# Mixing stage: 128-row transform tiles, an earlier split of the second weight, and a new order of norms and cosines

## What is computed

```python
def _moe_ref(x, w_ch1, w_ch2):
    X = np.fft.fft(x, axis=1)
    X = np.fft.fft(X, axis=2)
    mixed = np.real(X).astype(np.float32)
    u = x + mixed
    mu = np.mean(u, axis=-1, keepdims=True)
    var = np.mean((u - mu) ** 2, axis=-1, keepdims=True)
    un = (u - mu) / np.sqrt(var + 1e-06)
    ch = np.maximum(un @ w_ch1, 0.0) @ w_ch2
    return (u + ch).astype(np.float32)
```

## Time and profile before

| | |
|---|---|
| median of 3 runs | 956.68 us (956.54 to 957.53) |
| the profiled execution: its own time | 955.61 us |
| its span, first to last instruction | 953.5 us |
| mean granted TensorE clock | 0.912 |
| busy: PE, DVE, ACT, POOL | 90%, 49%, 33%, 21% |
| attention | to about 278 us |
| mixing | about 278 to 668 us |
| gated network | from about 671 us |

### The profile page before, as it was taken

How to read it: one execution, slowest core, us unless ns; L and a number is a source line. 1 busy time by engine, 2 the same in 40 slices (tenths; PEclk the granted TensorE clock), 3 DMA queues, 4 the chain that set the end, 5 groups by cost and what they waited for, 6 DMA issues and landing times. The chain is left out here.

```text
span 953.5 us, 24628 instructions
## 1 busy us (share of the span) xinstructions
PE 856.9 (90%) x10634; PEld 818.4 (86%) x10634; DVE 464.5 (49%) x1081; ACT 310.3 (33%) x665; POOL 201.1 (21%) x167
## 2 busy tenths in 40 slices
PE   6378888989877699999999999999689999999998
PEld 6378887889865589999999999999579989999897
DVE  4999976979163825333443243321472242342421
ACT  4246465674630302211122111111361241331421
POOL 3123213033001720800350000000032132232231
PEclk9757789797875889999999999999799999999999
DMA  9400514314335030022000101000532010000001
GB/s 376 128 34 29 188 58 159 106 40 151 121 103 170 1 112 7 17 67 66 8 17 17 57 17 50 27 10 17 173 106 67 33 41 33 25 0 25 26 1 50
DMA packets 31162, 65.13 MB, mean 68 GB/s; under 512 B 3482, under 2 KB 25315, under 8 KB 29539
## 3 DMA queue, kind: packets, MB, share of 16 engines
q1 hardware_dynamic: 31074, 63.85, 19.7%
HBM read 47.06 MB, written 14.16 MB: 64 GB/s over the span
## 5 line engine op out<-in xcount | busy, mean ns | idle before, releaser
L1039 PE MATMUL m_ps_h<-m_unt_hi,m_w_hi 128*128 128x256 f32 x432 | 122.7, 284 | 5.2 <-DVE m_h_lo L1220 3.2
L1039 PE MATMUL m_ps_h<-m_unt_hi,m_w_lo 128*128 128x256 f32 x432 | 121.9, 282 | 0.0
L1039 PE MATMUL m_ps_h<-m_unt_lo,m_w_hi 128*128 128x256 f32 x432 | 121.9, 282 | 0.0
L948 ACT ACTIVATE m_h_hi<-m_ps_h 128x512 fp32r<-128x512 f32 x72 | 43.1, 598 | 182.5 <-PE m_ps_h L1039 182.4
L1220 DVE SCALAR_TENSOR_TENSOR m_h_lo<-m_ps_h,m_h_hi 128x512 fp32r<-128x512 f32 x72 | 49.7, 691 | 99.5 <-ACT m_h_hi L948 99.3
L1039 PE MATMUL m_ps_d<-m_w_hi,m_h_hi 128*128 128x384 f32 x288 | 97.5, 338 | 0.0
L1039 PE MATMUL m_ps_d<-m_w_lo,m_h_hi 128*128 128x384 f32 x288 | 96.4, 335 | 0.0
L1039 PE MATMUL m_ps_d<-m_w_hi,m_h_lo 128*128 128x384 f32 x288 | 96.3, 334 | 0.0
L1039 PEld LDWEIGHTS m_ps_h<-m_unt_hi,m_w_hi 128*128 128x128 f32 x432 | 81.8, 189 | 6.0 <-DVE m_h_lo L1220 3.6
L1039 PEld LDWEIGHTS m_ps_h<-m_unt_hi,m_w_lo 128*128 128x128 f32 x432 | 82.9, 192 | 0.0
L1039 PEld LDWEIGHTS m_ps_h<-m_unt_lo,m_w_hi 128*128 128x128 f32 x432 | 82.2, 190 | 0.0
(11 more groups left out here) (205 smaller groups left out, 1960.5 us busy)
## 6 DMA issues: line engine op xcount, KB each, us to landing
kq<-kq_g SPq DMA_DIRECT2D x12, 1024.0 KB, 7.9
v_in<-v_g SPq DMA_DIRECT2D x6, 768.0 KB, 9.8
k_in<-k_g SPq DMA_DIRECT2D x6, 768.0 KB, 11.1
x_scr<-y_sb SPq DMA_DIRECT2D x24, 192.0 KB, 1.8
stage<-w_ch SPq DMA_DIRECT2D x6, 768.0 KB, 9.2
x_scr<-m_x_sb SPq DMA_DIRECT2D x24, 192.0 KB, 1.9
g_x<-x_scr SPq DMA_DIRECT2D x24, 192.0 KB, 3.5
out<-g_y SPq DMA_DIRECT2D x24, 192.0 KB, 1.9
```

The source lines that it names most:

```text
L948: act.activation(h_hi[:, 2 * g:2 * g + 2], ps_h[g % 2][:, :].rearrange("p (f t) -> p f t", f=2), ACT.Relu).then_inc(h_hi_ok, 1)
L1039: last = pe.matmul(out, first[x], second[y], start=(k == 0 and m == 0), stop=(k == n - 1 and m == 2))
```

## The change

All in `mixer`:

- **Spectrum**: every tile contracts 128 rows. The rows beyond 65 and 64 are zero in the tables, and the folds leave zero there.
- **Edge**: its two matmuls follow the columns of pair 0; in the batches DVE does `sums(b, 0)` ahead of `middle(b)`.
- **Chunk 3** is loaded with the first three, and DVE casts and subtracts it alone (`split`), after the folds. **Chunk 4** is loaded after the last token pieces of batch 0, ahead of three stores of the attention; ACT casts it between `sines(0, 0)` and `sines(0, 1)`, DVE subtracts it after `norm(0, 0)`. **Chunk 5** is loaded after the tokens of batch 0, ahead of those of batch 1; ACT casts it after group 0 of the hidden layer and DVE subtracts it after group 2.
- **Norm and fold**: `mirror(0, 1)`, `norm(0, 1)` and its root stand after the first hidden layer, and `fold_in(0)` waits for the first norm only.
- **Result**: tile 0 of pair 0 stands directly behind the hidden layer, in every batch, ahead of the next batch's spectrum ("next cosines") and the transpose. In the first pass it waits for each chunk of `w2` apart.

```diff
@@ sync
-            for c in range(DT):
+            for c in range(NS):
                 load_weights(sp, c)
...
             for place, source in token_pieces(0)[XE:XD]:
                 sp.dma_start(place, source).then_inc(x_in, 16)
+            sp.wait_ge(w_lo, 1)
+            load_weights(sp, NS)
...
             load_tokens(0)
-            load_weights(sp, DT)
+            sp.wait_ge(w_lo, 2)
+            load_weights(sp, NS + 1)
             sp.wait_ge(att["y_out"][1], 16 * last_group + 16)
             sp.wait_ge(x_free, 2)
             load_x(1)
-            for c in range(NS, WC):
-                sp.wait_ge(w_lo, c - NS + 1)
-                load_weights(sp, c)
@@ gpsimd
-            pool.wait_ge(un_ok, 2)
+            pool.wait_ge(un_ok, 1)
             fold_in(0)
@@ scalar
-                    if first and g % 2 == 0:
-                        weights(DT + g // 2)
+                    if first and g == 0:
+                        weights(WC - 1)
...
                 hidden(b, 0, first)
+                if first:
+                    roots(0, 1)
...
+            for q in att["y_out"]:
+                act.wait_ge(q, 16 * last_group + 16)
             sines(0, 0)
+            weights(NS)
             sines(0, 1)
             sines(0, 2)
             roots(0, 0)
             turned(0, 0)
-            roots(0, 1)
-            for q in att["y_out"]:
-                act.wait_ge(q, 16 * last_group + 16)
@@ tensor
-                            last = pe.matmul(ps[0:m, NK * c:NK * c + NK], x[0:ROWS[j], c, j], tab[0:ROWS[j], j],
+                            last = pe.matmul(ps[0:m, NK * c:NK * c + NK], x[:, c, j], tab[:, j],
                                              start=(j == tiles[0]), stop=(j == tiles[1]))
...
-            def result(b, r):
-                for c in range(2):
+            def result(b, r, *tiles):
+                for c in tiles:
                     pe.wait_ge(x2_ok, b * TT + (2 * r + c + 1))
                     for f in range(FT):
                         if c == 0 and f % 2 == 0:
                             pe.wait_ge(h_lo_ok, b * (R * HP) + (HP * r + f // 2 + 1))
+                        if r == 0 and c == 0 and f % 4 == 0:
+                            pe.wait_ge(w_lo, DT + f // 4 + 1)
...
                 hidden(b, 0)
+                result(b, 0, 0)
                 if not last_batch:
                     spectrum(b + 1, 0, ps_e, ps_o, False)
                 turn(b, 1)
-                pe.wait_ge(w_lo, WC)
-                result(b, 0)
+                result(b, 0, 1)
@@ vector
-                    if first and g % 2 == 0:
-                        weights(DT + g // 2)
+                    if first and g == 2:
+                        weights(WC - 1)
...
                 hidden(b, 0, first)
+                if first:
+                    mirror(0, 1)
+                    norm(0, 1)
+                results(b, 0, 0)
...
-                results(b, 0)
+                results(b, 0, 1)
...
                     dve.wait_ge(u_ok, b * R + 3)
+                    sums(b + 1, 0)
                     middle(b + 1)
-                    sums(b + 1, 0)
                     sums(b + 1, 1)
...
             folds(dve, FOLDS, fold_dve, slice(2, KT))
+            dve.wait_ge(att["y_done"], att["steps"])
+            split(DT)
             spectrum(0, 0, ps_e, True)
             spectrum(0, 1, ps_h[0], True)
+            sums(0, 0)
             middle(0)
-            sums(0, 0)
             sums(0, 1)
             mirror(0, 0)
             norm(0, 0)
+            weights(NS)
             dve.wait_ge(u_ok, 1)
             sums(0, 2)
             turned(0, 0)
-            mirror(0, 1)
-            norm(0, 1)
             batch(0, True, False)
```

## The result

| | before | after |
|---|---|---|
| median | 956.61 us (955.28 to 957.53, 4 runs) | 940.36 us (938.53 to 943.43, 4 runs) |
| profiled execution, its span | 955.61, 953.5 us | 938.53, 936.4 us |
| mean granted TensorE clock | 0.912 | 0.918 |

The ratio is 0.9831, 95% interval 0.9813 to 0.9848: 16 us faster. A second measurement of the same kernel, on the same chip as the second group of experiments, gave 942.43 us (939.59 to 943.4) and 0.9855 (0.9828 to 0.9882). The forecast was 939.4, range 936.5 to 945.0. One execution of the whole study, 977.28 us at a mean granted clock of 0.798, fell in a slower state of the chip and is left out everywhere.

The account below looks back on a forecast made before the run. TensorE, busy 90% of the span, was taken as the bound, behind a serial first chain. Terms summed to -13.3 us (943.4); a chosen -4.0 for an early clock rise made -17.3 us, 939.4, range 936.5 to 945.

Parts of the forecast that it names:

- Rows and early clock: First batch's transforms: 128 rows remove 64-row gaps, -1.7 us; gapless work raises the clock early, -4.0 us.
- The chosen term: First transforms: without gaps the clock rises 3 to 4.7 us in; -4.0 us, counted by choice.
- Rival 1: First transforms: the clock stays low there, giving 943.4 us (942 to 944.5); chance 0.28.
- Edge, first batch: First batch's second columns wait for first columns, ACT's copy, two sums and the edge copy; +0.85 us.
- First hidden layer: First pass: two weight subtractions and the norm leave, PE's first wait goes, a 1.2 us wait comes; -2.0 us.
- Fold and clock behind it: First pass: PE's wait for POOL's fold goes, -4.2 us; the low clock behind it goes, -3.7 and -0.9 us.
- Second norm: DVE, moved behind the first hidden layer: done between 333 and 335 us, PE wants it at 335; cost 0.
- rival 2: Second norm late: DVE and POOL block each other, PE waits 3 to 8 us at its transpose; 947 us, chance 0.08.
- rival 3: Transforms: the gap is not the row count, so no row gains and no early clock rise; 949.4 us, chance 0.05.
- Weights: Second weight's chunks 3 to 5, loaded and split at new places, hidden behind other waits; cost 0.
- Rival 4: Moved weight loads delay the next batch's tokens on SP's queue, PE stands before its transform; 960 us, chance 0.02.
- The edge order: Later batches: the edge copy stands behind two sums, 0.54 us later, three times; +1.6 us.

Follow-up runs that it names:

- rows_undone: Changed kernel with 65 and 64 rows restored in the transform tiles; 951.53 us, ratio 0.9939.
- rows_first: Kernel before with 128-row transform tiles in the first batch's two spectra only; 950.19 us against 957.82, ratio 0.9910.
- rows_65: Changed kernel with the third and fourth transform tiles contracting 65 rows each; 943.4 us against the changed kernel's 942.43.
- result_whole: Changed kernel with both result tiles of a first pair behind the transpose again, in every batch; 949.04 us, ratio 0.9932.
- edge_first: Changed kernel with edge matmuls and the copy of their row back ahead of first columns and sums, all batches; 936.37 us, ratio 0.9782.
- norm_fold_old: Changed kernel with the second norm back ahead of the first hidden layer and the fold waiting for it again; 944.97 us.
- norm_ahead: Changed kernel with mirror, norm and root of the second pair back ahead of the first hidden layer, fold still early; 953.75 us.
- rows_only: Kernel before with one edit, all four transform tiles contracting 128 rows; 942.87 us against 957.3, ratio 0.9856.
- edge_early: Changed kernel with edge matmuls behind the second hidden layer (first batch: ahead of first columns), their copy earlier on DVE; 932.79 us, again 932.82.

## Why the prediction was right, and where its terms were not

From the first transform to the second hidden layer it was 357.49 - 282.99 = 74.5 us and is 339.94 - 282.81 = 57.1 us: 17.4 less, where the terms of this stretch add up to 16.3.

- **Rows and early clock.** From the first transform to the first columns' matmuls (the edge pair before), 14.29 us became 9.13: -5.2, forecast -1.7 - 4.0. The chosen term was right: `rows_undone` has no early rise, `rows_first` has it. Rival 1 is out. With the scatter of that stretch the term is worth 4.1 to 5.7 us from profile to profile.
- **Edge, first batch.** From there to the third columns 4.26 us became 4.37: +0.1, forecast +0.85. At the low clock the order costs about what it should: in `rows_undone` the same stretch is 5.27 us, 1.0 more than before. In the changed kernel the first columns run at the high clock, which pays for it; I had left that gain out as "up to 1.8 more".
- **First hidden layer.** 334.01 - 311.97, less the fold's 4.2, is 17.9 us; now 321.11 - 306.73 = 14.4: -3.5, forecast -2.0. The 1.2 us wait I expected before the sixth group did not come. The step that did not hold here is that the subtraction that is left "finds POOL in an operation". DVE and POOL of the kernel after:

```profile
316.23 2.06 DVE L1125 TENSOR_TENSOR m_w_lo<-stage,m_w_hi 128x1536 fp32r<-128x1536 f32 x1
316.64 3.37 POOL L766 TENSOR_TENSOR m_x_in_sb<-m_half 128x768 f32<-128x768 f32 x1
```

DVE's subtraction issued ahead of POOL's operation, and POOL waited instead (3.37 us for a piece that takes 1.8). The mechanism itself is right. In `rows_65`, `result_whole`, `edge_first` and `norm_fold_old` the same subtraction takes 2.97, 3.14, 3.29 and 3.72 us, and PE waits 0.8, 0.8, 1.0 and 1.4 us for `h_lo`. Which of the two comes first is decided by a few tenths.
- **Fold and clock behind it.** The wait is gone (-4.2). The fold's cosines are done at 322.2 and needed at 327.36: 5 us to spare, where I had 6. From the spectrum or first result to the end of the second result, 20.32 us became 16.35 (321.11 to 337.46): -4.0, forecast -4.6, with 0.36 us of new wait for `un` in it.
- **Second norm.** Forecast 0, measured 0.4 at its place. The mechanism of rival 2 is there at small size. DVE of the kernel after:

```profile
322.55 1.90 DVE L1175 TENSOR_TENSOR m_u<-m_x_tok,m_ppq 128x193 f32<-128x193 f32 x1
324.37 1.99 DVE L1176 TENSOR_TENSOR m_u<-m_x_tok,m_pmq 128x191 f32<-128x191 f32 x1
```

Two additions of 0.35 us take 1.9 and 2.0 beside POOL's of 322.38 and 324.19. The Trainium skill ("SBUF — State Buffer", Practical consequences) has the later of two such instructions blocked until the other is done; these rows and `norm_ahead` agree. In `norm_ahead` TENSOR_SCALAR operations with one SBUF tensor operand (310.82, 317.12) were held too. The same section of the Trainium skill lists `tensor_scalar` among the operations that can contend with GpSimd, under conditions on its operands; my count of operations "with two operands in SBUF" left them out.
- **Second spectrum's sines.** 3.16 us became 2.48: -0.7, as forecast; rival 3 is out, by `rows_only` too.
- **Weights.** Forecast 0 at their new places. The cast and subtraction of chunk 3 (284.77 to 287.53) end 0.6 us before DVE's next input; that of chunk 4 (303.03 to 304.78) stands in the hole before `turned`. Rival 4's mechanism is there at small size: the token loads of batch 1 begin 4.6 us behind the first transform instead of 3.5, POOL stands idle for 1.3 us before its fold at 307.80, and the queue moves data up to about 307.3. The profile names no releaser for that wait, so that the tokens end it is inferred. It costs nothing here, with 5 us to spare at the cosines.
- **Batches 1 to 3.** Four more spectra halves 4 x 0.67 = -2.7, as forecast. The edge order 3 x 0.52 = +1.6, as forecast. Two things were not in the sum: the clock fell twice (+3.2), and the hidden layer behind the sine transform went quicker three times: it took 352.34 - 339.94 = 12.40 us instead of 370.35 - 357.49 = 12.86: -1.4.

Together -17.4 + 1.6 - 2.7 + 3.2 - 1.4 = -16.7 us up to the last result, where the forecast had -17.3. The last result starts 16.97 us earlier (638.27 instead of 655.24), 0.2 of it because the first transform did. So the mechanisms of the large terms were right, and the closeness of the total is in part luck: the falls of the clock, +3.2 us, stood in no term, and the first hidden layer (1.5 better than forecast), the quicker later hidden layers (1.4) and the first batch's edge order (0.75) happened to pay for them. My +1.6 for the edge order was the wrong price of a right mechanism. I had priced the clock behind the wait for the fold, and did not do so for the edge waits, where I even listed a clock of 1.00 up to the stage's end as a sign. With the falls the order costs 4.8 us in this profile. `edge_first` gives back 3.1 us of B, with one fall left, and `edge_early` 8.0, since it takes the old 0.8 us waits away too.

The Trainium skill's advice to tile rows for short contractions ("TensorEngine Tiling (Array Packing)", Row Tiling) was weighed as the rule against this change. The rows decided rightly: with nothing in a second row tile, the 64-row matmul among longer ones costs 0.66 us per four matmuls at the high clock, and 65 rows cost nothing.

## What to carry to other kernels

A wait of PE can be dearer than it reads: price the clock behind it as well, and ask first for a place where its producer can go a whole phase earlier, which here took two matmuls and one small copy. Look at the number of rows where PE shows gaps between short matmuls: 64 rows among 128-row tiles were dearer here than 65 or 128. And keep a chain of small dependent VectorE operations away from long GpSimd ones in SBUF, since it can wait out a GpSimd operation at each link; here half of such a move (the fold earlier, the norm at its old place) cost 9 us, and the whole of it gained 1 to 3.

## What the runs showed of the hardware that I had not expected

- A PE wait of 1.5 us in a stream of matmuls was followed by the low clock in 19 of 24 cases, a wait of 0.8 us in 1 of 12. The two profiles of the changed kernel have it at the same two places.
- The 108 matmuls of a hidden layer directly behind a sine spectrum took 12.86 us where that spectrum had 64-row matmuls, and 12.4 to 12.5 where it had 65 or 128. Behind results they took 12.72, in all kernels. The matmuls themselves start 113, 118 or 119 ns apart. What sets this pace was not tried and stays open.
- Moving one wait number of POOL, beside the norm's old place, changed the time by 9 us (953.75 and 944.97).
